# One core, a gated and a plain feed-forward stage: the low odd weights of two d_ff tiles share one pass of half-row matmuls

## What is computed

```python
B, H, S, D = 2, 8, 768, 40            # attention; B * S = 1536 tokens, d_model = H * D = 320
C = f * C + i * outer(v_t, k_t);  n = f * n + i * k_t
y[t] = sigmoid(o_t) * (C @ q_t) / max(abs(n . q_t), 1)      # a gated recurrence, t = 0 .. 767

xn = x / sqrt(mean(x * x) + 1e-6) * rms_g                   # x: [1536, 320]
g = xn @ w_gate                                             # d_ff = 1536
x2 = (g * sigmoid(g) * (xn @ w_val)) @ w_out

h = x2 @ w_in                                               # d_ff = 2048
out = maximum(0.01 * h, h) @ w_out2
```

## Time and profile before

| what | value |
|---|---|
| median of 3 runs | 473.02 us (472.62 to 473.37) |
| profiled execution | 474.08 us, span 472.3 us |
| mean granted clock of TensorE | 0.988 |
| TensorE busy (matmuls) | 448.3 us, 2722 instructions |
| VectorE busy | 263.0 us |
| ScalarE busy | 179.8 us |
| GpSimd busy | 103.8 us |

### The profile page before, as it was taken

How to read it: one execution, slowest core, us unless ns; L and a number is a source line. 1 busy time by engine, 2 the same in 40 slices (tenths; PEclk the granted TensorE clock), 3 DMA queues, 4 the chain that set the end, 5 groups by cost and what they waited for, 6 DMA issues and landing times.

```text
span 472.3 us, 7154 instructions
## 1 busy us (share of the span) xinstructions
PE 448.3 (95%) x2722; PEld 411.4 (87%) x2722; DVE 263.0 (56%) x492; ACT 179.8 (38%) x350; POOL 103.8 (22%) x95
## 2 busy tenths in 40 slices
PE   2669998999999999999999999999999999999997
PEld 1669988899999999999888888799889989988996
DVE  7556788676657787666553333733434333453434
ACT  1464543434232343242433322655334343333332
POOL 2469649302113032000122210352000000000000
PEclk9987999999999999999999999999999999999999
DMA  5868363303122142200032210230000000010101
GB/s 164 288 201 261 118 202 108 117 7 113 37 81 78 41 119 70 95 1 0 2 92 62 62 32 0 61 93 0 1 0 1 1 1 0 1 57 0 57 0 56
DMA packets 21439, 31.64 MB, mean 67 GB/s; under 512 B 1328, under 2 KB 15296, under 8 KB 21408
## 3 DMA queue, kind: packets, MB, share of 16 engines
q1 hardware_dynamic: 21408, 31.22, 21.5%
HBM read 29.20 MB, written 2.02 MB: 66 GB/s over the span
## 4 chain that ended last, share of the span: by engine, by line
PE 85%; DVE 6%; issue 3%; ACT 2%; DMA 2%; POOL 1%; SPq 0%; DVEq 0%; POOLq 0%; ACTq 0%
PE gate_ps L949 23%; PE value_ps L949 22%; PE out_ps L978 9%; PE out_ps L1015 8%; PE out_ps L982 3%; PE even_ps L1015 3%; PE c_ps L1015 3%; PE odd_ps L1015 3%; PE odd_ps L924 3%; PE even_ps L924 2%; PE c_ps L914 2%; DMA expo<-decay_scratch 1%; PE even_ps L892 1%; PE odd_ps L903 1%; PE odd_ps L892 1%
## 5 line engine op out<-in xcount | busy, mean ns | idle before, releaser
L768 DVE TENSOR_TENSOR h_lo<-hid,h_hi 128x512 fp32r<-128x512 f32 (+2 forms) x96 | 73.3, 763 | 62.1 <-ACT h_hi L502 62.1
L502 ACT ACTIVATE h_hi<-hid 128x512 fp32r<-128x512 f32 (+2 forms) x96 | 55.5, 579 | 120.1 <-DVE hid L755 81.8
L949 PE MATMUL gate_ps<-x_hi,w_sb 128*128 128x512 f32 (+2 forms) x288 | 70.6, 367 | 2.5 <-DVE act_buf L749 1.5
L949 PE MATMUL value_ps<-x_hi,w_sb 128*128 128x512 f32 (+2 forms) x288 | 69.9, 365 | 0.0
L949 PEld LDWEIGHTS gate_ps<-x_hi,w_sb 128*128 128x128 f32 x288 | 49.3, 192 | 8.6 <-issue 2.3
L949 PEld LDWEIGHTS value_ps<-x_hi,w_sb 128*128 128x128 f32 x288 | 49.7, 192 | 4.3
L490 ACT ACTIVATE act_buf<-gate_ps 128x384 f32<-128x384 f32 (+2 forms) x48 | 23.4, 487 | 75.3 <-PE gate_ps L949 75.2
L978 PE MATMUL out_ps<-h_hi,w_sb 128*128 128x384 f32 (+2 forms) x192 | 49.1, 340 | 1.6 <-DVE h_lo L768 1.6
L749 DVE SCALAR_TENSOR_TENSOR act_buf<-act_buf,gate_ps 128x384 f32<-128x384 f32 (+2 forms) x48 | 26.5, 552 | 38.9 <-ACT act_buf L490 38.9
L393 POOL TENSOR_TENSOR w_sb<-raw,w_sb 128x704 fp32r<-128x704 f32 x16 | 27.4, 1715 | 76.8 <-ACT w_sb L484 76.8
L1015 PE MATMUL out_ps<-w_sb,h_hi 128*128 128x320 f32 x192 | 42.8, 308 | 0.0
(11 more groups left out here) (170 smaller groups left out, 818.2 us busy)
## 6 DMA issues: line engine op xcount, KB each, us to landing
raw<-in_w SPq DMA_DIRECT2D x12, 544.0 KB, 5.1
att_sb<-in_tok SPq DMA_DIRECT2D x12, 512.0 KB, 4.7
expo<-decay_scratch SPq DMA_DIRECT2D x12, 512.0 KB, 6.0
raw<-in_w SPq DMA_DIRECT2D x16, 352.0 KB, 2.9
att_sb<-in_qk SPq DMA_DIRECT2D x24, 160.0 KB
out_y<-y_acc SPq DMA_DIRECT2D x12, 160.0 KB, 1.9
consts_sb<-in_consts SPq DMA_DIRECT2D x1, 129.5 KB, 2.4
gates_sb<-in_gates SPq DMA_DIRECT2D x1, 96.0 KB, 2.4
```

Of the source, the lines that this page charges most:

```text
L502: nc.scalar.activation(h_hi[:, r, 0:n], hid[:, r, 0:n], ACT.Copy).then_inc(hi_done, 1)
L768: nc.vector.tensor_tensor(h_lo[:, r, 0:n], hid[:, r, 0:n], h_hi[:, r, 0:n].bitcast(F32), ALU.subtract).then_inc(h_done, 1)
L949: last = nc.tensor.matmul(ps[:, 0:n], lhs, rhs, start=(j == 0), stop=(j == len(xs) - 1))
```

## The change

The matmul with the low odd weights needs only rows 0 to 63 (low weights times the high part of x). The change takes it out of `in_product` (7 matmuls are left) and lets two d_ff products share one pass: `low_odd` issues a matmul on rows 0 to 63 into the first bank and one on rows 64 to 127 into the second bank, directly behind each other. In phase 1 the two are gate and value of one step, in phase 2 the tiles f and f + 1 (f even). The high odd matmul stays a whole one. For the half on rows 64 to 127 the high part of x is needed there too: a new buffer `x_odd2`, written by VectorE in `x_low` and `x2_odd`. The order of the columns of a weight tile changes, and the low odd weights of gate and value go into one block of 128 columns, rows 0 to 63 for gate and 64 to 127 for value, by two instructions of 64 rows.

```diff
@@ lo_weights (GpSimd); lo_first (VectorE) likewise, without the waits
-                    nc.gpsimd.tensor_tensor(w[:, LO1:LO1 + W1M], r[:, 0:W1M],
-                                            w[:, 0:W1M].bitcast(F32), ALU.subtract)
+                    nc.gpsimd.tensor_tensor(w[:, LO1:LO1 + WHOLE1], r[:, 0:WHOLE1],
+                                            w[:, 0:WHOLE1].bitcast(F32), ALU.subtract).then_inc(lo_whole, 1)
+                    pool.wait_ge(lo_whole, i + 1 if i < DVE_W else i)
+                    for z in range(2):
+                        rows, odd = slice(z * HP, (z + 1) * HP), slice(WHOLE1 + z * P, WHOLE1 + (z + 1) * P)
+                        ins = nc.gpsimd.tensor_tensor(w[rows, LO1 + WHOLE1:W1], r[rows, odd],
+                                                      w[rows, odd].bitcast(F32), ALU.subtract)
+                    ins.then_inc(lo_odd, 1)
+                    pool.wait_ge(lo_odd, i + 1 if i < DVE_W else i)
@@ x_low
-                    op0=ALU.mult, op1=ALU.subtract).then_inc(x_done, 1)
+                    op0=ALU.mult, op1=ALU.subtract)
+                nc.vector.tensor_copy(x_odd2[ODD:P, tok], x_odd[0:ODD, tok].bitcast(F32)).then_inc(x_done, 1)
@@ x2_odd
                 dve.wait_ge(x2_taken, KT * (c + 1))
+                nc.vector.tensor_copy(x_odd2[ODD:P, cols], tail[:, 0:n])
                 then(nc.vector.tensor_copy(x_odd[0:ODD, cols], tail[:, 0:n]))
@@ in_product
-                      (part(2, 0), x_odd[:, cols]), (part(2, 1), x_odd[:, cols])]
+                      (part(2, 0), x_odd[:, cols])]
@@ new
+            def low_odd(first_ps, first_w, second_ps, second_w, cols, n):
+                last = nc.tensor.matmul(first_ps[:, 0:n], first_w[0:ODD, :], x_odd[0:ODD, cols],
+                                        start=False, stop=True)
+                nc.tensor.matmul(second_ps[:, 0:n], second_w[ODD:P, :], x_odd2[ODD:P, cols],
+                                 start=True, stop=False)
+                return last
@@ gate
-                in_product(gate_ps, w1_sb[:, f, :], 0, LO1, cols1(c), TILES1[c] * P,
-                           tiles=FIRST if s == 0 else 0).then_inc(in_done, 1)
+                in_product(gate_ps, w1_sb[:, f, :], 0, WHOLE1, LO1, cols1(c), TILES1[c] * P, False,
+                           tiles=FIRST if s == 0 else 0)
+                pe.wait_ge(hid_done, after(s - 1))
+                low = w1_sb[:, f, LO1 + WHOLE1:W1]
+                low_odd(gate_ps, low, value_ps, low, cols1(c), TILES1[c] * P).then_inc(in_done, 1)
@@ value
-                pe.wait_ge(hid_done, after(s - 1))
-                in_product(value_ps, w1_sb[:, f, :], KT * P, LO1, cols1(c), TILES1[c] * P)\
+                in_product(value_ps, w1_sb[:, f, :], 2 * P, WHOLE1 + P, LO1, cols1(c), TILES1[c] * P, True)\
                     .then_inc(in_done, 1)
@@ in2
+                last = in_product(in_ps[f % 2], w[:, f, :], 0, 2 * P, W2RAW, cols, CHUNK, f % 2 == 1)
+                if f % 2 == 0:
+                    pe.wait_ge(hid_done, after(s - 1))
+                    if c == 0:
+                        wait_lo(pe, NF1 + g * GF + f + 1)
+                    low = slice(W2RAW + 2 * P, W2RAW + 3 * P)
+                    last = low_odd(in_ps[0], w[:, f, low], in_ps[1], w[:, f + 1, low], cols, CHUNK)
```

More of the change, by code:

```diff
@@ L69 @@
 TOK = ATT - V0
-W1M = 2 * KT * P + 2 * P
+WHOLE1 = 6 * P
+W1M = WHOLE1 + 2 * P
 W1RAW = W1M + ODD
-W1 = 2 * W1RAW
 LO_ODD = W1RAW
 LO1 = W1RAW + ODD
+W1 = LO1 + WHOLE1 + P
 W2RAW = KT * P + DM
@@ L108, in build @@
         x_odd = sb(ctx, "x_odd", [P, TILES * P], F32R)
+        x_odd2 = sb(ctx, "x_odd2", [P, TILES * P], F32R)
         raw = sb(ctx, "raw", [P, RAW, W1RAW])
@@ L216, in build @@
         w_lo = sem("w_lo")
+        lo_whole = sem("lo_whole")
+        lo_odd = sem("lo_odd")
         first_sum = sem("first_sum")
@@ L632, in lo_first @@
                 w, r = w1_sb[:, i, :], raw[:, i % RAW, :]
-                nc.vector.tensor_tensor(w[:, LO1:LO1 + W1M], r[:, 0:W1M], w[:, 0:W1M].bitcast(F32),
+                nc.vector.tensor_tensor(w[:, LO1:LO1 + WHOLE1], r[:, 0:WHOLE1], w[:, 0:WHOLE1].bitcast(F32),
                                         ALU.subtract)
+                for z in range(2):
+                    rows, odd = slice(z * HP, (z + 1) * HP), slice(WHOLE1 + z * P, WHOLE1 + (z + 1) * P)
+                    nc.vector.tensor_tensor(w[rows, LO1 + WHOLE1:W1], r[rows, odd], w[rows, odd].bitcast(F32),
+                                            ALU.subtract)
                 nc.vector.tensor_tensor(w[:, LO_ODD:LO_ODD + ODD], r[:, W1M:W1RAW],
@@ L935, in turn, with in_product @@
                 nc.tensor.transpose(turned_ps(n)[0:ODD, 2 * P:3 * P], x[:, 2 * P:DM], ident_sb).then_inc(t_done, 1)
-            def in_product(ps, w, c0, lo, cols, n, tiles=0):
+            def in_product(ps, w, c0, odd, lo, cols, n, second, tiles=0):
                 def part(k, low):
-                    start = c0 + k * P + (lo if low else 0)
+                    start = (odd if k == 2 else c0 + k * P) + (lo if low else 0)
                     return w[:, start:start + P]
@@ L948, in in_product @@
                         pe.wait_ge(x_done, tiles)
-                    last = nc.tensor.matmul(ps[:, 0:n], lhs, rhs, start=(j == 0), stop=(j == len(xs) - 1))
+                    last = nc.tensor.matmul(ps[:, 0:n], lhs, rhs, start=(j == 0 and not second),
+                                            stop=(second and j == len(xs) - 1))
+                return last
[4 more added lines that the diff above has]
+                                 start=True, stop=False)
                 return last
@@ L971, in out1 @@
                 w = w1_sb[:, f, :]
-                o, r, n = 2 * KT * P, s % 2, TILES1[c] * P
+                o, r, n = 4 * P, s % 2, TILES1[c] * P
                 for k in range(2):
@@ L995, in in2 @@
                 pe.wait_ge(hid_done, after(s - 2))
-                in_product(in_ps[s % 2], w2_sb[g][:, f, :], 0, W2RAW, slice(c * CHUNK, (c + 1) * CHUNK), CHUNK)\
-                    .then_inc(in_done, 1)
+                w, cols = w2_sb[g], slice(c * CHUNK, (c + 1) * CHUNK)
+                last = in_product(in_ps[f % 2], w[:, f, :], 0, 2 * P, W2RAW, cols, CHUNK, f % 2 == 1)
[5 more added lines that the diff above has]
+                    last = low_odd(in_ps[0], w[:, f, low], in_ps[1], w[:, f + 1, low], cols, CHUNK)
+                last.then_inc(in_done, 1)
             def out2(s, g, c, f):
@@ L1109, in in_rows @@
         return stacked.reshape(KT, P, n, P).transpose(2, 1, 0, 3).reshape(n, P, KT * P)
-    w1 = np.concatenate([in_rows(np.asarray(moe_w_gate)), in_rows(np.asarray(moe_w_val)),
-                         np.asarray(moe_w_out).reshape(NF1, P, DM)], axis=2)
+    gate, val, w_out = in_rows(np.asarray(moe_w_gate)), in_rows(np.asarray(moe_w_val)), \
+        np.asarray(moe_w_out).reshape(NF1, P, DM)
+    w1 = np.concatenate([gate[:, :, 0:2 * P], val[:, :, 0:2 * P], w_out[:, :, 0:2 * P],
+                         gate[:, :, 2 * P:], val[:, :, 2 * P:], w_out[:, :, 2 * P:]], axis=2)
     w2 = np.concatenate([in_rows(np.asarray(moe2_w_in)), np.asarray(moe2_w_out).reshape(NF2, P, DM)], axis=2)
```

## The result

| | before | after |
|---|---|---|
| median | 473.19 us (472.62 to 473.57, 4 runs) | 489.13 us (487.12 to 489.74, 4 runs) |
| profiled execution, its span | 474.08, 472.3 us | 488.87, 487.1 us |
| ratio to before | | 1.0331 (1.0312 to 1.035) |

The change costs 15.9 us. It was forecast at 489.5 us, 16.5 more than before.

The account below looks back on a forecast made before the run. TensorE's back-to-back stream was taken to bound the kernel from chunk 1 on, chunk 0 being mixed. 14.1 + 2.2 + 1.2 - 1.0 = + 16.5 us gave 490.6 profiled, 489.5 us as median; range 483 to 494.

Parts of the forecast that it names:

- The halves run together: Each pair on TensorE costs one pass instead of two, in phases 1 and 2: 14.0 us saved.
- The price of a stay: Going into half rows and out on TensorE costs 0.39 us, 72 times; net of saved passes + 14.1 us.
- Rivals 1, 2 and 3: 1: free entry, 461.8 us, chance 0.09; 2: only one side costs, 475.5, 0.06; 3: halves do not overlap, 503.5, 0.05.
- The start: Start of phase 1: VectorE's two `x_low` copies wait for GpSimd, making `x_done` late: + 2.2 us.
- The forward wait: Chunk 0, steps 6 and 9: `hid_done` is waited for ahead of the low pair, 0.6 us each, + 1.2 us.
- What chunk 0 absorbs: Part of chunk 0's 3.3 us of switches falls where TensorE waited anyway: - 1.0 us, bounds 0 and - 3.3.
- GpSimd's longer low part: A tile's low part becomes four instructions, 0.6 us more per tile; covered by 1.1 us at tile 9, so nothing.

Follow-up runs that it names:

- the last version: Kernel before, with the shared low odd pair directly behind `scores` only in 7 steps of 384 columns, ScalarE copying token tiles 2 to 7: 472.02 us, ratio 0.9967.

## Why the prediction was right, point by point

**The halves run together, also at 512 columns.** Both start at 264.65, and leaving one out changed nothing (488.82 against 489.13).

**The price of a stay.** I read 0.39 us from `scores`; the stream shows 0.38. The 512-column steps of phase 1 went from 5.57 to 5.73 us (+ 0.16, forecast + 0.156), two steps of phase 2 from 7.21 to 7.39 (+ 0.18, forecast + 0.16), and chunks 1 and 2 grew by 4.9 us for 24 steps (forecast 5.2). That it is the pair was shown by the two whole matmuls (- 11.1 us) and that it is the row halves by 64 against 96 rows (21.3 us). Rivals 1, 2 and 3 fell with these: the entry is not free, both sides cost, the halves overlap.

**The start.** The two copies came out as described; TensorE waited 1.9 us for the second, and the fifth matmul of the first gate stood 3.05 us behind the first instead of 1.02, 2.0 us more (forecast 2.2). With the copies on ScalarE 2.6 us went, of which part is the forward wait below.

**The forward wait.** It stands twice in chunk 0, 1.3 and 0.8 us, 2.1 in all. I had 0.6 each, 1.2 in the sum, although my own parts (0.3, and 0.4 to 0.7 for the copy) make 0.7 to 1.0. With the copy on ScalarE the two waits are 0.2 and 0.5 us, and in the changed kernel the copies in front of them took 1.18 and 0.84 us. So the term was undersized, and by the copy.

**What chunk 0 absorbs.** It was undersized too, in the other direction. Chunk 0 was to grow by 3.3 + 2.2 + 1.2 - 1.0 = 5.7 us and grew by 4.1, although the waits were longer than I had put them. Some of the waits that it had before are gone: TensorE's for `h_lo` (1.6 us) is no longer in the list, and that for the gate fell from 1.5 to 0.3. I treated chunk 0 as a stream with some slack. It is a loop over TensorE, ScalarE and VectorE, and in it the granted clock is not the same from run to run, which my sum had only in its high end: it was back at 1.00 at 44.4 us in the changed kernel, 41.3 before, 36.8 with two whole matmuls, 45.0 with 96 rows and 35.3 in the last version. How much of the 4.1 us is clock I can only bound: the stretch at half the clock was 3.4 us longer than before (30.8 to 44.4 us against 31.1 to 41.3), which costs at most 1.7 us (an estimate), and the last version, at full clock 6 us earlier than before, has a chunk 0 of the same length (59.2 us against 59.3). Four experiments missed their numbers in part by what chunk 0 did (two whole matmuls, 96 rows, the pair behind scores, the pair twice); which share is the clock's and which the loop's is open.

**What was missing.** The sum had no term for the third instruction of `x2_odd`, which costs 0.7 us at the start of phase 2. By stage, 5.7 us were forecast for chunk 0, 5.2 for chunks 1 and 2, 1.9 for chunk 3 and 3.7 for phase 2, and 4.1, 4.9, 1.9 and 4.9 came. The forward waits were too small by 0.9, the absorption by more than 2, and this was missing; the errors cancelled. The mechanism and the price of a stay were right, but that the total came within 0.6 us (15.9 against 16.5) is luck.

**GpSimd's longer low part** was priced at nothing. No wait of TensorE for low weights appears in the changed kernel. But where the stream of chunk 0 is shorter they do appear: 0.5 us with two whole matmuls, 1.0 with 96 rows, 1.2 with two whole matmuls and the copy on ScalarE. So the cover sufficed in the changed kernel, and not where TensorE's stream was shorter. I did not try the longer low part alone.

## What to carry to other kernels

Sharing one pass between two half-row matmuls saves a pass and costs a stay: about 0.38 us here at full clock, with 256, 384 and 512 columns. In the trace the loads on the way in and on the way out start with their matmuls, not a pass ahead, and each side stands 0.09 to 0.10 us late besides; that the array runs empty there is my reading of it. Group half-row work so that a stay saves at least two passes of 512 columns (three of 384), or put it beside half-row work that is there already; a single pair among whole matmuls loses at all three widths. And look through the kernel before for the same form of instruction: how early and how late its neighbours start prices the change before it is built.

## What the runs showed of the hardware that I had not expected

A half-row matmul on its own pays as much as a pair: 488.82 us with one half, 489.13 with both. A matmul on 96 rows pays nothing, and neither does one that writes 64 of 128 output rows. At the slow clock (granted 0.50, 1.2 GHz) a stay costs more, by the timeline of the first step: the pair starts 0.34 us behind a pass whose usual distance is 0.21, and 0.51 us pass from it to the next whole one.
